# Normalising on VectorE instead of TensorE, finishing each down sum by halves, three tanh units begun at once, and the last stores on two queues, in a fused attention and two-layer feed-forward kernel on one core

## The chip, the cores and the metric

One core of one Trainium2 chip runs the kernel. The metric is device time in microseconds (us). Three runs of the kernel before gave 1197.57 us as median (1196.62 to 1197.73). Engines are named as in the profile: PE is TensorE (PEld its weight loads), DVE VectorE, ACT ScalarE, POOL GpSimd, SP SyncE; SPq and ACTq are the queues from which those engines issue transfers.

## The reference

6016 tokens of 256 channels go through a channel attention and two feed-forward layers.

```python
qn = q / (norm(q, axis=1) + 1e-6);  kn = k / (norm(k, axis=1) + 1e-6)
a = softmax(kn.T @ qn / tau)                 # 256 x 256, sums over all tokens
x = v @ a                                    # 6016 x 256
xn = x / sqrt(mean(x * x, axis=-1) + 1e-6) * rms_g
g, val = xn @ w_gate, xn @ w_val             # 256 -> 1536
y = (g * sigmoid(g) * val) @ w_out           # 1536 -> 256
h = y @ w_in                                 # 256 -> 2048
out = (h - tanh(h)) @ w_out2                 # 2048 -> 256
```

## The kernel before, in words

A first part streams q and k through PE in pieces of rows, builds the 256 x 256 attention matrix and normalises it. Then come twelve tiles of 512 tokens, the last of 384. Everything in a tile is kept with channels on the 128 partitions and tokens along the row. Tile 0 is written out by itself, tiles 1 to 9 are a hardware loop, tiles 10 and 11 are written out again.

Every fp32 factor is split into a rounded high part and a low rest, so one product is three matmuls (`PASSES`, L302): high by high, high by low, low by high. A tile has two stages. The first has G = 12 gated units of 128 hidden channels: gate and value are made by `up` (six matmuls each: two halves c of the 256 inputs by three passes), ACT applies the sigmoid, DVE multiplies twice (L718, L721), rounds (L819) and takes the rest (L731, result `h_lo`), and `down` adds the unit into the two halves d of `y_acc` (again six matmuls). The second stage has H = 16 tanh units: one `up` each, ACT tanh (L480), DVE subtracts (L727), L819, L731, and `down` adds into `out_acc`.

PE's order is written by hand (L964 to L1007). A unit's `down` comes LAG = 3 units behind its `up`; behind the last `up` of a stage stand four `down`s in a row (24 matmuls): one from the loop and three from the loop at L986 or L1006. Each `down` waits for `h_ready`, which `h_lo` counts. The matmul results of `up` go through a ring of four PSUM banks. At the end of a stage ACT copies `y_acc` rounded into `y_hi` (L501) and DVE makes `y_lo` (L738), half by half: half 0 may start at `y_full`, which is counted when half 0's last matmul is done, three matmuls before the stage's end (L955), half 1 when all is done. The first tanh unit waits for half 0 and then for half 1 (`y_ready`). In tiles 1 to 10 the next tile's x is made in between (`make_x`, twelve matmuls, L991); in tile 0 and in the last tile nothing stands there.

The norm of the next tile's x is made along the tanh units, by a table of unit numbers (L38, `next_x` L741): squares added (L584), transposed by blocks of 32 (L589), reduced (L593, giving `sums`, 128 x 16, where each quadrant of 32 partitions holds a part of each token's sum), the four quadrants added by one matmul with the constant matrix `quads` (`add_quads`, L919), the root on ACT (L424), the reciprocal and its spreading on DVE (L599, L601). In tile 0 the first x is normalised while PE already computes the first three gated units from x without the norm (`raw_gate`, `raw_value`, L755 to L766); there `add_quads` stands inside the first value unit (`sum_first`, L959), and everything DVE does next waits for it through ACT's root.

`quads` is filled by POOL (L396 to L402) behind its share of the weight splitting; `CONSTANTS` counts that fill, and DVE waits for it at L668 before it turns the norms of q and k into reciprocals (L671). Behind that stand the softmax and tile 0. PE runs matmuls without use at two places there (`warm_up`, L1009).

The results are transposed by DVE (L621, one instruction for each half of the channels) and stored by eight transfers per tile from SPq, four for each half (`store`, L337). ACTq is used for three loads at the start only (L432).

Of the kernel before, what the change touches and what calls it, by code (L numbers as in the profile page):

```python
# [5 lines left out]
F32 = mybir.dt.float32  # L6
# [5 lines left out]
P = 128  # L12
# [3 lines left out]
LAG = 3  # L16
RING = 4
# [18 lines left out]
SUM_AT = 4  # L36
SQRT_AT = 5
X_ADD, X_TURN, X_REDUCE, X_RMS, X_SCALE, X_CAST, X_SPLIT = 0, 1, 2, 6, 7, 9, 10  # L38
# [12 lines left out]
def build(nc, q, k, v, tau, w_gate, w_value, w_down, w_up2, w_down2, rms_g, out):  # L51
# [62 lines left out]
    with ExitStack() as ctx:  # L114
# [9 lines left out]
        quads = sb("quads", [P, P], F32)  # L124
# [34 lines left out]
        sums = sb("sums", [P, TILE // SQ], F32)  # L159
        rms = sb("rms", [P, TILE // SQ], F32)  # L160
# [37 lines left out]
        token_sums = y_acc[:, 0, 0:TILE // SQ]  # L198
# [36 lines left out]
        sum_step = sem("sum_step")  # L235
        sums_full = sem("sums_full")
# [16 lines left out]
        stored = sem("stored")  # L253

# [55 lines left out]
        def _(sp):  # L310
# [60 lines left out]
            sp.wait_ge(stored, TILE_DMAS * TILES)  # L371
# [3 lines left out]
        def _(pool):  # L375
# [20 lines left out]
            nc.gpsimd.memset(quads[:], 0.0).then_inc(constants, 1)  # L396
            for n in range(2 * QUADS - 1):

                pool.wait_ge(constants, 4 + n)
                nc.gpsimd.affine_select(out=quads[:], in_=quads[:], compare_op=ALU.not_equal, fill=1.0,  # L400
                                        base=(n - (QUADS - 1)) * SQ, pattern=[[-1, P]],
                                        channel_multiplier=1).then_inc(constants, 1)  # L402


        @block.scalar
        def _(act_e):
# [15 lines left out]
            def root(t, width):  # L422
                act_e.wait_ge(sums_full, t + 1)
# [135 lines left out]
            tile(TILES - 1, True)  # L559


        @block.vector
        def _(dve):
# [27 lines left out]
            def reduce_squares(t, width):  # L591
# [3 lines left out]
                                        AX_X, ALU.add).then_inc(sum_step, 1)  # L595

# [71 lines left out]
            dve.wait_ge(constants, CONSTANTS)  # L668
# [42 lines left out]
            reduce_squares(0, TILE)  # L711
            spread_scales(0, TILE)
# [28 lines left out]
            def next_x(t, f, ahead):  # L741
# [4 lines left out]
                if f == X_REDUCE:  # L746
                    reduce_squares(t + 1, ahead)
                if f == X_RMS:
                    spread_scales(t + 1, ahead)
# [98 lines left out]
        def _(pe):  # L848
# [70 lines left out]
            def add_quads(t, width):  # L919

                pe.wait_ge(sum_step, t * SUM_STEPS + SUM_STEPS)
                nc.tensor.matmul(token_sums[:, 0:width // SQ], quads[:, :], sums[:, 0:width // SQ],  # L922
                                 start=True, stop=True).then_inc(sums_full, 1)

            def tile(t, first, last):
# [3 lines left out]
                def up(name, weights, hi, lo, made=None, between=None):  # L929

                    free_bank(t, name)
                    for c in range(KC):
                        if made is not None:
                            pe.wait_ge(*made(c))
                        if c > 0 and between is not None:
                            between()
                        for w_part, part in PASSES:
                            ins = nc.tensor.matmul(bank(name)[:, 0:width], weights(c, w_part),  # L938
                                                   (hi if part else lo)[:, c, 0:width],
                                                   start=c == 0 and w_part and part,  # L940
                                                   stop=c == KC - 1 and not w_part)
                    ins.then_inc(bank_full, 1)

                def down(kind, f, u, units, acc, full):

                    if first and f % (BLOCK // C) == 0:
                        pe.wait_ge(w_ready, place[(kind, f // (BLOCK // C))] + 1)
                    pe.wait_ge(h_ready, t * U + (u + 1))
                    for d in range(KC):
                        for w_part, part in PASSES:  # L950
                            ins = nc.tensor.matmul(acc[:, d, 0:width], down_weight(kind, f, d, w_part),  # L951
                                                   (h_hi if part else h_lo)[:, u % RING, 0:width],
                                                   start=f == 0 and w_part and part,
                                                   stop=f == units - 1 and not w_part)
                        if f == units - 1 and d == 0:  # L955
                            ins.then_inc(full, 1)
                    ins.then_inc(h_used, 1)

                def sum_first():  # L959
                    pe.wait_ge(constants, CONSTANTS)  # L960
                    pe.wait_ge(x_copied, KC)
                    add_quads(0, TILE)

                for f in range(G):  # L964
# [3 lines left out]
                    for which, name in ((0, "gate"), (1, "value")):  # L968
# [3 lines left out]
                        if f == (RAW_UNITS if first else 0):  # L972
                            made = lambda c: (x_ready, t * KC + (c + 1))
                        up((name, f), lambda c, part: gv_weight(which, f, c, part),
                           u_hi if raw_unit else x_hi, u_lo if raw_unit else x_lo, made,
                           sum_first if first and (name, f) == ("value", 0) else None)

                    for late in ((), (0, 1))[f == LAG + 1] if first and f <= LAG + 1 else (f - LAG,):
                        if late < 0:
                            continue  # L980
                        if late == 0:
                            pe.wait_ge(rms_ready, t + 1)
                            if not first:
                                pe.wait_ge(y_ready, t * KC)
                        down("down", late, late, G, y_acc, y_full)
                for f in range(G - LAG, G):  # L986
                    down("down", f, f, G, y_acc, y_full)
# [4 lines left out]
                for f in range(H):  # L992
# [80 lines left out]
```

## Time and profile before

| | value |
|---|---|
| median of 3 runs | 1197.57 us |
| the profiled execution | 1195.46 us |
| its span (first to last instruction) | 1193.3 us |
| granted TensorE clock, mean | 0.998 |
| busy: PE, PEld | 99%, 83% |
| busy: DVE, ACT, POOL | 71%, 31%, 2% |
| chain that ended last: PE's share | 95% |

The span is what the trace covers; the rest of the execution's time lies around it. Busy shares are of the span. The chain that ended last goes back from the last instruction to whatever released it. PE's matmuls are pipelined: the listed duration of one (0.39 us) holds its way through the array, and the next starts some 0.23 us after it.

### The profile page before, as it was taken

Reading aid. Unit: us, or ns where it says so; the run is one execution under the profiler, and the core shown is the slowest. Engines: PE = TensorE matmul, PEld = TensorE weight load, DVE = VectorE, ACT = ScalarE, POOL = GpSimd, SP = SyncE. Lnnn points to the kernel's source line nnn. Section 1 sums busy time; section 2 is a strip of 40 time slices with the busy share of each in tenths; the row PEclk is TensorE's granted clock in tenths of the full one; section 3 lists DMA queues with packets and bytes.
Section 4 is the critical chain, followed back from the end, with each engine's and each line's share of the span. In section 5 each row is a group of like instructions: output and inputs, shape, how many; then the busy total and the mean of one; then the engine's idle time right before and its main releaser. Section 6 shows DMA issues by size and latency. Waiting matters only on the chain.

```text
span 1193.3 us, 15914 instructions
## 1 busy us (share of the span) xinstructions
PE 1179.2 (99%) x5339; PEld 986.0 (83%) x5339; DVE 845.0 (71%) x1375; ACT 365.9 (31%) x587; POOL 29.3 (2%) x27
## 2 busy tenths in 40 slices
PE   8999999999999999999999999999999999999998
PEld 7777888888888888888888888888888888888997
DVE  5697766866767677586596676766767758658665
ACT  6765621411321322231231141142132123123121
POOL 4400000000000000000000000000000000000000
PEclk9999999999999999999999999999999999999999
DMA  9515011011002002002001101100200100100100
GB/s 344 211 62 151 1 18 18 1 18 18 0 2 33 0 0 35 0 0 35 0 0 18 18 0 18 18 0 0 35 0 0 31 0 0 18 1 1 18 1 14
DMA packets 105210, 33.92 MB, mean 28 GB/s; under 512 B 92384, under 2 KB 100832, under 8 KB 105184
## 3 DMA queue, kind: packets, MB, share of 16 engines
q1 hardware_dynamic: 104752, 33.05, 11.0%
q10 hardware_dynamic: 432, 0.52, 0.1%
q8 instruction: 16, 0.26, 0.1%
q14 instruction: 10, 0.08, 0.0%
HBM read 27.40 MB, written 6.16 MB: 28 GB/s over the span
## 4 chain that ended last, share of the span: by engine, by line
PE 95%; DMA 2%; DVE 1%; POOL 1%; ACT 0%; SPq 0%; issue 0%; POOLq 0%; DVEq 0%; ACTq 0%
PE ring L938 54%; PE out_acc L951 21%; PE y_acc L951 16%; PE out_acc L909 2%; DMA qk_in<-in_q_dram 2%; PE y_acc L855 1%; PE y_acc L866 1%; POOL we_lo L393 0%; SPq L319 0%; PE y_acc L922 0%; PE y_acc L909 0%; POOL quads L400 0%; ACT y_hi L471 0%; DVE y_lo L738 0%; PE out_acc L1031 0%
## 5 line engine op out<-in xcount | busy, mean ns | idle before, releaser
L480 ACT ACTIVATE act<-ring 128x512 f32<-128x512 f32 (+1 forms) x333 | 196.5, 590 | 715.4 <-PE ring L938 698.9
L731 DVE TENSOR_TENSOR h_lo<-act,h_hi 128x512 fp32r<-128x512 f32 (+1 forms) x336 | 228.6, 680 | 10.7
L727 DVE TENSOR_TENSOR act<-ring,act 128x512 f32<-128x512 f32 (+1 forms) x192 | 129.2, 673 | 99.3 <-ACT act L480 99.2
L718 DVE TENSOR_TENSOR act<-ring,act 128x512 f32<-128x512 f32 (+1 forms) x141 | 94.9, 673 | 140.9 <-ACT act L480 140.9
L938 PE MATMUL ring<-y_hi,wl_hi 128*128 128x512 f32 (+1 forms) x384 | 148.8, 388 | 1.7 <-DVE y_lo L738 1.7
L938 PE MATMUL ring<-y_lo,wl_hi 128*128 128x512 f32 (+1 forms) x384 | 147.8, 385 | 0.0
L938 PE MATMUL ring<-y_hi,wl_lo 128*128 128x512 f32 (+1 forms) x384 | 147.7, 385 | 0.0
L951 PE MATMUL out_acc<-h_hi,wl_hi 128*128 128x512 f32 (+1 forms) x384 | 147.6, 384 | 0.0
L951 PE MATMUL out_acc<-h_lo,wl_hi 128*128 128x512 f32 (+1 forms) x384 | 147.6, 384 | 0.0
L951 PE MATMUL out_acc<-h_hi,wl_lo 128*128 128x512 f32 (+1 forms) x384 | 147.6, 384 | 0.0
L819 DVE CAST h_hi<-act 128x512 fp32r<-128x512 f32 (+1 forms) x308 | 129.8, 421 | 12.9
L938 PE MATMUL ring<-x_hi,wl_hi 128*128 128x512 f32 (+1 forms) x288 | 110.7, 384 | 0.0
L938 PE MATMUL ring<-x_lo,wl_hi 128*128 128x512 f32 (+1 forms) x288 | 110.7, 384 | 0.0
L938 PE MATMUL ring<-x_hi,wl_lo 128*128 128x512 f32 (+1 forms) x288 | 110.7, 384 | 0.0
L721 DVE TENSOR_TENSOR act<-ring,act 128x512 f32<-128x512 f32 (+1 forms) x141 | 95.9, 680 | 15.4
L938 PE MATMUL ring<-x_hi,we_hi 128*128 128x512 f32 (+1 forms) x276 | 106.2, 385 | 0.1
L938 PE MATMUL ring<-x_lo,we_hi 128*128 128x512 f32 (+1 forms) x276 | 106.1, 384 | 0.0
L938 PE MATMUL ring<-x_hi,we_lo 128*128 128x512 f32 (+1 forms) x276 | 106.1, 384 | 0.0
L938 PEld LDWEIGHTS ring<-y_hi,wl_hi 128*128 128x128 f32 x384 | 72.1, 188 | 15.8 <-issue 2.4
L951 PEld LDWEIGHTS out_acc<-h_hi,wl_hi 128*128 128x128 f32 x384 | 72.1, 188 | 14.0 <-DVE h_lo L731 0.2
L938 PEld LDWEIGHTS ring<-y_hi,wl_lo 128*128 128x128 f32 x384 | 72.1, 188 | 13.8
L951 PEld LDWEIGHTS out_acc<-h_hi,wl_lo 128*128 128x128 f32 x384 | 72.1, 188 | 13.7
(156 smaller groups left out, 1596.7 us busy)
## 6 DMA issues: line engine op xcount, KB each, us to landing
out_dram<-out_rows SPq DMA_DIRECT2D x88, 64.0 KB, 1.8
qk_in<-in_k_dram SPq DMA_DIRECT2D x9, 512.0 KB, 9.6
qk_in<-in_q_dram SPq DMA_DIRECT2D x9, 512.0 KB, 10.4
v_in<-in_v_dram SPq DMA_DIRECT2D x72, 64.0 KB, 2.2
w_in<-in_moe_w_out_dram SPq DMA_DIRECT2D x14, 256.0 KB, 2.9
w_in<-in_moe_w_in_dram SPq DMA_DIRECT2D x8, 256.0 KB, 3.2
w_in<-in_moe_w_gate_dram SPq DMA_DIRECT2D x6, 256.0 KB, 6.3
w_in<-in_moe_w_val_dram SPq DMA_DIRECT2D x6, 256.0 KB, 7.1
```

The costliest lines, as they stand in the source:

```text
L480: nc.scalar.activation(act[:, u % RING, 0:width], bank(name)[:, 0:width], func).then_inc(act_ready, 1)
L718: nc.vector.tensor_tensor(buf, bank(gate)[:, 0:width], buf, ALU.mult).then_inc(bank_free, 1)
L721: nc.vector.tensor_tensor(buf, bank(value)[:, 0:width], buf, ALU.mult).then_inc(bank_free, 1)
L727: nc.vector.tensor_tensor(buf, bank(hidden)[:, 0:width], buf, ALU.subtract).then_inc(bank_free, 1)
L731: nc.vector.tensor_tensor(h_lo[:, u % RING, 0:width], act[:, u % RING, 0:width], f32(h_hi[:, u % RING, 0:width]), ALU.subtract).then_inc(h ...
L819: nc.vector.tensor_copy(h_hi[:, slot, 0:width], act[:, slot, 0:width]).then_inc(h_hi_ready, 1)
L855: ins = nc.tensor.matmul(raw[:, m, 0:C], qk_in[:, stage, 0, j, m * P:(m + 1) * P], qk_in[:, stage, 1, j, :], start=i == 0 and j == 0, stop ...
L866: ins = nc.tensor.matmul(raw[:, m, 0:C], (qk_hi if k_part else qk_lo)[:, s % SLOTS, 0, j, m * P:(m + 1) * P], (qk_hi if q_part else qk_lo) ...
L909: ins = nc.tensor.matmul(acc[:, d, 0:width], (a_hi if a_part else a_lo)[:, c, d * P:(d + 1) * P], (hi if v_part else lo)[:, c, 0:width], s ...
L938: ins = nc.tensor.matmul(bank(name)[:, 0:width], weights(c, w_part), (hi if part else lo)[:, c, 0:width], start=c == 0 and w_part and part ...
L951: ins = nc.tensor.matmul(acc[:, d, 0:width], down_weight(kind, f, d, w_part), (h_hi if part else h_lo)[:, u % RING, 0:width], start=f == 0 ...
```

## The change

Four things are changed.

1. The four quadrants' partial sums are added by DVE. `quads`, POOL's fill of it and PE's `add_quads` go; DVE gets a function of that name with two adds of 64 partitions and four of 32, whose second input lies in another quadrant than the first. In tile 0 it stands behind the reduce, in the others behind the tanh unit of number 3 (`X_QUADS`). The softmax on DVE then waits for `ident` only.
2. The last three `down`s of each stage are done half by half: half 0 of all three units, then half 1 (`finish_down`).
3. In tile 0 and in the last tile the first three tanh units are begun together: half 0 of the inputs for all three, then half 1 (`hidden_units`, `HIDDEN_BEGUN`). In tiles 1 to 10 it is one unit, as before.
4. The last half of the last tile is stored by two transfers from SPq and two from ACTq.

```diff
-SUM_AT = 4
-X_ADD, X_TURN, X_REDUCE, X_RMS, X_SCALE, X_CAST, X_SPLIT = 0, 1, 2, 6, 7, 9, 10
+X_ADD, X_TURN, X_REDUCE, X_QUADS, X_RMS, X_SCALE, X_CAST, X_SPLIT = 0, 1, 2, 3, 6, 7, 9, 10
...
@@ store (SP) @@
-                    for quad in range(QUADS):
+
+                    shared = isinstance(t, int) and t == TILES - 1 and half == KC - 1
+                    for quad in range(QUADS // 2 if shared else QUADS):
...
@@ scalar @@
-                act_e.wait_ge(sums_full, t + 1)
+                act_e.wait_ge(sums_full, (t + 1) * QUADS)
...
+            act_e.wait_ge(out_turned, TILES * KC)
+            for quad in range(QUADS // 2, QUADS):
+                act_e.dma_start(tokens(out, TILES - 1, SHORT, KC - 1, quad),
+                                out_rows[quad * SQ:(quad + 1) * SQ, KC - 1, 0:SHORT // SQ, :]).then_inc(stored_last, 16)
@@ vector @@
+            def add_quads(t, width):
+
+                dve.wait_ge(sum_step, t * SUM_STEPS + SUM_STEPS)
+                for a in range(2):
+                    here, there = slice(a * 2 * SQ, (a + 1) * 2 * SQ), slice((1 - a) * 2 * SQ, (2 - a) * 2 * SQ)
+                    nc.vector.tensor_tensor(pair_sums[here, 0:width // SQ], sums[here, 0:width // SQ],
+                                            sums[there, 0:width // SQ], ALU.add).then_inc(pairs_ready, 1)
+                dve.wait_ge(pairs_ready, (t + 1) * 2)
+                for a in range(QUADS):
+                    here, there = slice(a * SQ, (a + 1) * SQ), slice((a ^ 1) * SQ, ((a ^ 1) + 1) * SQ)
+                    nc.vector.tensor_tensor(token_sums[here, 0:width // SQ], pair_sums[here, 0:width // SQ],
+                                            pair_sums[there, 0:width // SQ], ALU.add).then_inc(sums_full, 1)
...
-            dve.wait_ge(constants, CONSTANTS)
+            dve.wait_ge(constants, IDENT)
@@ tensor @@
+                def down_half(kind, f, d, u, units, acc):
+                    for w_part, part in PASSES:
+                        ins = nc.tensor.matmul(acc[:, d, 0:width], down_weight(kind, f, d, w_part),
+                                               (h_hi if part else h_lo)[:, u % RING, 0:width],
+                                               start=f == 0 and w_part and part,
+                                               stop=f == units - 1 and not w_part)
+                    return ins
...
+                def finish_down(kind, u, units, acc, full):
+
+                    for f in range(units - LAG, units):
+                        pe.wait_ge(h_ready, t * U + (u + f + 1))
+                        ins = down_half(kind, f, 0, u + f, units, acc)
+                    ins.then_inc(full, 1)
+                    for f in range(units - LAG, units):
+                        down_half(kind, f, 1, u + f, units, acc).then_inc(h_used, 1)
+
+                def hidden_units(units):
+
+                    for f in units:
+                        free_bank(t, ("hidden", f))
+                    for c in range(KC):
+                        pe.wait_ge(y_ready, t * KC + (c + 1))
+                        for f in units:
+                            up_half(("hidden", f), c, lambda c, part: up2_weight(f, c, part), y_hi, y_lo)
...
-                for f in range(G - LAG, G):
-                    down("down", f, f, G, y_acc, y_full)
+                finish_down("down", 0, G, y_acc, y_full)
...
+                begun = HIDDEN_BEGUN if first or last else 1
+                hidden_units(range(begun))
+                for f in range(begun, H):
...
-                    if f == SUM_AT and not last:
-                        add_quads(t + 1, ahead)
-                for f in range(H - LAG, H):
-                    down("down2", f, G + f, H, out_acc, out_full)
+                finish_down("down2", G, H, out_acc, out_full)
```

PE at the end of the second stage of the loop (tiles 1 to 9), before: the units numbered 14 and 15, from the rows that follow unit 13's `down`. `out_acc` is the sum of the stage, `wl_hi` and `wl_lo` the weight parts.

```order
L948 REGISTER_ALU
L951 MATMUL out_acc<-h_hi,wl_hi 128x512 [waits h_ready]
L951 MATMUL out_acc<-h_lo,wl_hi 128x512
L951 MATMUL out_acc<-h_hi,wl_lo 128x512
L951 MATMUL out_acc<-h_hi,wl_hi 128x512
L951 MATMUL out_acc<-h_lo,wl_hi 128x512
L951 MATMUL out_acc<-h_hi,wl_lo 128x512
L948 REGISTER_ALU
L951 MATMUL out_acc<-h_hi,wl_hi 128x512 [waits h_ready]
L951 MATMUL out_acc<-h_lo,wl_hi 128x512
L951 MATMUL out_acc<-h_hi,wl_lo 128x512
L951 MATMUL out_acc<-h_hi,wl_hi 128x512
```

And PE there now, from the first of the three last units (13) on.

```order
L975 REGISTER_ALU
L958 MATMUL out_acc<-h_hi,wl_hi 128x512 [waits h_ready]
L958 MATMUL out_acc<-h_lo,wl_hi 128x512
L958 MATMUL out_acc<-h_hi,wl_lo 128x512
L975 REGISTER_ALU
L958 MATMUL out_acc<-h_hi,wl_hi 128x512 [waits h_ready]
L958 MATMUL out_acc<-h_lo,wl_hi 128x512
L958 MATMUL out_acc<-h_hi,wl_lo 128x512
L975 REGISTER_ALU
L958 MATMUL out_acc<-h_hi,wl_hi 128x512 [waits h_ready]
L958 MATMUL out_acc<-h_lo,wl_hi 128x512
L958 MATMUL out_acc<-h_hi,wl_lo 128x512
```

Before, six matmuls stood between the wait for one unit and the wait for the next; now three do. The nine matmuls of half 1 follow behind these rows.

PE at the start of the last tile's tanh units, before: the first unit's two halves with their waits for `y_ready`, then the second unit.

```order
L938 MATMUL ring<-y_hi,wl_hi 128x384 [waits y_ready,bank_free]
L938 MATMUL ring<-y_lo,wl_hi 128x384
L938 MATMUL ring<-y_hi,wl_lo 128x384
L938 MATMUL ring<-y_hi,wl_hi 128x384 [waits y_ready]
L938 MATMUL ring<-y_lo,wl_hi 128x384
L938 MATMUL ring<-y_hi,wl_lo 128x384
L938 MATMUL ring<-y_hi,wl_hi 128x384 [waits bank_free]
L938 MATMUL ring<-y_lo,wl_hi 128x384
L938 MATMUL ring<-y_hi,wl_lo 128x384
```

And now: half 0 of three units, then the wait for half 1.

```order
L942 MATMUL ring<-y_hi,wl_hi 128x384 [waits bank_free,y_ready]
L942 MATMUL ring<-y_lo,wl_hi 128x384
L942 MATMUL ring<-y_hi,wl_lo 128x384
L942 MATMUL ring<-y_hi,wl_hi 128x384
L942 MATMUL ring<-y_lo,wl_hi 128x384
L942 MATMUL ring<-y_hi,wl_lo 128x384
L942 MATMUL ring<-y_hi,wl_hi 128x384
L942 MATMUL ring<-y_lo,wl_hi 128x384
L942 MATMUL ring<-y_hi,wl_lo 128x384
L942 MATMUL ring<-y_hi,wl_hi 128x384 [waits y_ready]
L942 MATMUL ring<-y_lo,wl_hi 128x384
L942 MATMUL ring<-y_hi,wl_lo 128x384
```

Three matmuls stood between the wait for half 0 and the wait for half 1; now nine do, and the first unit is complete after twelve instead of six.

DVE in tile 0, before, from the adding of the squares to the spreading of the reciprocals.

```order
L584 TENSOR_TENSOR vt<-vt 128x512 [waits sq_ready]
L589 STREAM_TRANSPOSE scales<-vt 128x512 [waits sum_step]
L593 TENSOR_REDUCE sums<-scales 128x16 [waits sum_step]
L599 RECIPROCAL rrms<-rms 128x16 [waits rms_ready]
L601 STREAM_TRANSPOSE scales<-rrms 128x512 [waits scale_step]
```

And now, with two rows more at the end.

```order
L585 TENSOR_TENSOR vt<-vt 128x512 [waits sq_ready]
L590 STREAM_TRANSPOSE scales<-vt 128x512 [waits sum_step]
L594 TENSOR_REDUCE sums<-scales 128x16 [waits sum_step]
L603 TENSOR_TENSOR pair_sums<-sums 64x16 [waits sum_step]
L603 TENSOR_TENSOR pair_sums<-sums 64x16
L608 TENSOR_TENSOR token_sums<-pair_sums 32x16 [waits pairs_ready]
L608 TENSOR_TENSOR token_sums<-pair_sums 32x16 x3
L613 RECIPROCAL rrms<-rms 128x16 [waits rms_ready]
L615 STREAM_TRANSPOSE scales<-rrms 128x512 [waits scale_step]
```

Six adds now stand ahead of the reciprocal, and ACT's root waits for the last of them.

SP's last rows before: each half of the last tile is one transfer that waits and three more.

```order
L341 DMA out_0_dram<-out_rows 32x16x32 [waits out_turned]
L341 DMA out_0_dram<-out_rows 32x16x32 x3
L341 DMA out_0_dram<-out_rows 32x12x32 [waits out_turned]
L341 DMA out_0_dram<-out_rows 32x12x32 x3
L341 DMA out_0_dram<-out_rows 32x12x32 [waits out_turned]
L341 DMA out_0_dram<-out_rows 32x12x32 x3
L114 UNCONDITIONAL_BRANCH [waits stored]
```

And now.

```order
L345 DMA out_0_dram<-out_rows 32x16x32 [waits out_turned]
L345 DMA out_0_dram<-out_rows 32x16x32 x3
L345 DMA out_0_dram<-out_rows 32x12x32 [waits out_turned]
L345 DMA out_0_dram<-out_rows 32x12x32 x3
L345 DMA out_0_dram<-out_rows 32x12x32 [waits out_turned]
L345 DMA out_0_dram<-out_rows 32x12x32
L114 UNCONDITIONAL_BRANCH [waits stored_last,stored]
```

Two of the eight are gone from here; they stand at the end of ACT's program, behind its last tanh, and wait for the same transpose.

## Rows read from the trace of the kernel before

**Rows 1.** The page: busy time of the engines.
```profile
PE 1179.2 (99%) x5339; PEld 986.0 (83%) x5339; DVE 845.0 (71%) x1375; ACT 365.9 (31%) x587; POOL 29.3 (2%) x27
```
**Rows 2.** Busy time in the stretch of one tile of the loop.
```profile
159.46:255.16 95.70, 95.70 (x424) 78.98 (x423) 68.07 (x111) 25.14 (x42) 0.00 (x0) 1.00 0.07 12
```
**Rows 3.** The chain that ended last, in order of time: start, us, what.
```profile
219.46 1.36 PE out_acc L951 x6
220.82 0.38 PE y_acc L922 x2
221.20 1.48 PE ring L938 x6
...
1081.54 0.12 PE y_acc L922 x2
```
**Rows 4.** Instructions in order: start, duration, engine; last `up` matmul, last `h_lo`, loop tile.
```profile
249.49 0.39 PE L938 MATMUL ring<-y_hi,wl_lo 128*128 128x512 f32 x1
...
251.90 0.69 DVE L731 TENSOR_TENSOR h_lo<-act,h_hi 128x512 fp32r<-128x512 f32 x1
```
**Rows 5.** The same view, tile 0: PE released by an `h_lo`.
```profile
79.25 0.68 DVE L731 TENSOR_TENSOR h_lo<-act,h_hi 128x512 fp32r<-128x512 f32 x1
...
79.98 0.50 PE L951 MATMUL y_acc<-h_hi,we_hi 128*128 128x512 f32 x1
```
**Rows 6.** The same, first stage's end, loop tile: last `h_lo`, last of 24 matmuls.
```profile
204.62 0.69 DVE L731 TENSOR_TENSOR h_lo<-act,h_hi 128x512 fp32r<-128x512 f32 x1
...
208.19 0.39 PE L951 MATMUL y_acc<-h_hi,wl_lo 128*128 128x512 f32 x1
```
**Rows 7.** The same, ahead of the softmax; in brackets idle time and what ended it.
```profile
52.57 0.17 ACT L456 ACTIVATE norms<-out_acc 128x4 f32<-128x4 f32 x1 [2.11 <-PE out_acc L895]
...
53.83 0.16 DVE L671 SCALAR_TENSOR_TENSOR norms<-norms,tau 128x4 f32<-128x4 f32 x1 [3.36 <-POOL quads L400]
...
52.40 1.91 PE L1012 MATMUL ring<-vt_hi 128*128 128x512 f32 x4
54.78 1.22 PE L1031 MATMUL out_acc<-act,ones 128*128 128x256 f32 x2 [0.47 <-DVE act L676]
```
**Rows 8.** The same, the first norm in tile 0.
```profile
65.89 0.69 DVE L593 TENSOR_REDUCE sums<-scales 128x16 f32<-128x512 f32 x1
...
67.12 0.27 ACT L424 ACTIVATE rms<-y_acc,eps 128x16 f32<-128x16 f32 x1 [1.37 <-PE y_acc L922]
...
67.43 0.25 DVE L599 RECIPROCAL rrms<-rms 128x16 f32<-128x16 f32 x1 [0.86 <-ACT rms L424]
...
81.72 0.50 PE L938 MATMUL ring<-x_hi,we_hi 128*128 128x512 f32 x1
```
**Rows 9.** The same, tile 0 between its stages.
```profile
111.66 0.68 DVE L731 TENSOR_TENSOR h_lo<-act,h_hi 128x512 fp32r<-128x512 f32 x1
...
115.53 0.47 PE L938 MATMUL ring<-y_hi,wl_hi 128*128 128x512 f32 x1 [0.88 <-DVE y_lo L738]
...
119.80 0.68 DVE L731 TENSOR_TENSOR h_lo<-act,h_hi 128x512 fp32r<-128x512 f32 x1
...
121.08 0.39 PE L951 MATMUL out_acc<-h_hi,wl_hi 128*128 128x512 f32 x1
```
**Rows 10.** The same, last tile: its first tanh unit, its last `h_lo`.
```profile
1154.06 0.41 PE L938 MATMUL ring<-y_hi,wl_hi 128*128 128x384 f32 x1 [0.80 <-DVE y_lo L738]
...
1185.00 0.56 DVE L731 TENSOR_TENSOR h_lo<-act,h_hi 128x384 fp32r<-128x384 f32 x1
```
**Rows 11.** The last stores and the first loads of ACTq; the last wait.
```profile
1187.12 1.11 DVE L621 STREAM_TRANSPOSE out_rows<-out_acc 128x384 f32<-128x384 f32 x2 [1.57 <-PE out_acc L951]
1187.73 3.90 SPq L341 DMA_DIRECT2D out_dram<-out_rows  x8
...
0.74 1.39 ACTq L432 DMA_DIRECT2D qk_in<-in_q_dram  x3
...
SPq L114 <- DMA out_dram<-out_rows: 1.3, 1, 1.3
```

More of the change, by code:

```diff
@@ L16 @@
 LAG = 3
+HIDDEN_BEGUN = 3
 RING = 4
@@ L747, in next_x @@
                     reduce_squares(t + 1, ahead)
+                if f == X_QUADS:
+                    add_quads(t + 1, ahead)
                 if f == X_RMS:
@@ L927, in tile, with up_half, up @@
                 ahead = width_of(t + 1)
-                def up(name, weights, hi, lo, made=None, between=None):
+                def up_half(name, c, weights, hi, lo):
+                    for w_part, part in PASSES:
+                        ins = nc.tensor.matmul(bank(name)[:, 0:width], weights(c, w_part),
+                                               (hi if part else lo)[:, c, 0:width],
+                                               start=c == 0 and w_part and part,
+                                               stop=c == KC - 1 and not w_part)
+                    if c == KC - 1:
+                        ins.then_inc(bank_full, 1)
+                def up(name, weights, hi, lo, made=None):
                     free_bank(t, name)
@@ L934, in up, with down @@
                             pe.wait_ge(*made(c))
[L935 to L944, printed above, removed]
+                        up_half(name, c, weights, hi, lo)
+                def down_half(kind, f, d, u, units, acc):
+                    for w_part, part in PASSES:
+                        ins = nc.tensor.matmul(acc[:, d, 0:width], down_weight(kind, f, d, w_part),
[3 more added lines that the diff above has]
+                    return ins
+                def down(kind, f, u, units, acc):
                     if first and f % (BLOCK // C) == 0:
@@ L949, in down @@
                     for d in range(KC):
[L950 to L956, printed above, removed]
-                    ins.then_inc(h_used, 1)
[L959 to L962, printed above, removed]
+                        ins = down_half(kind, f, d, u, units, acc)
+                    ins.then_inc(h_used, 1)
+                def finish_down(kind, u, units, acc, full):
[12 more added lines that the diff above has]
+                            up_half(("hidden", f), c, lambda c, part: up2_weight(f, c, part), y_hi, y_lo)
                 for f in range(G):
@@ L981, in tile @@
                         if late == 0:
-                            pe.wait_ge(rms_ready, t + 1)
-                            if not first:
+                            if first:
+                                pe.wait_ge(x_copied, KC)
+                            else:
                                 pe.wait_ge(y_ready, t * KC)
-                        down("down", late, late, G, y_acc, y_full)
-                for f in range(G - LAG, G):
-                    down("down", f, f, G, y_acc, y_full)
+                        down("down", late, late, G, y_acc)
+                finish_down("down", 0, G, y_acc, y_full)
                 if not last and not first:
@@ L991, in tile @@
                     make_x(x_acc, vt_hi, vt_lo, ahead, WHOLE_X)
-                for f in range(H):
+                if first:
+                    pe.wait_ge(w_ready, place[("up2", 0)] + 1)
+                begun = HIDDEN_BEGUN if first or last else 1
+                hidden_units(range(begun))
+                for f in range(begun, H):
                     if first and f % (BLOCK // KC // P) == 0:
                         pe.wait_ge(w_ready, place[("up2", f // (BLOCK // KC // P))] + 1)
-                    up(("hidden", f), lambda c, part: up2_weight(f, c, part), y_hi, y_lo,
-                       (lambda c: (y_ready, t * KC + (c + 1))) if f == 0 else None)
+                    up(("hidden", f), lambda c, part: up2_weight(f, c, part), y_hi, y_lo)
                     if f >= LAG:
```

26 lines of the change are left out of this document (9 added, 17 removed).

## Prediction

> **What bounds the kernel.** I read the page's busy times first: PE is busy for 99% of the span [rows 1]. So only what leaves PE's own stream, or what holds it at its few gaps, can move the time. The stretch of one loop tile says more: PE is busy through all of its 95.70 us with 424 matmuls, at a granted clock of 1.00, that is 2.4 GHz [rows 2]. The chain of waits in order of time gives the price of a matmul: six take 1.36 us, 0.2267 each [rows 3]. 420 such matmuls are 95.20 us; the remaining 0.50 us of a tile belongs to the four records that are not of that kind or that stand beside it, and the chain names them: 0.38 us for the sum over the quadrants and 0.12 more in the six behind it (1.48 for 1.36) [rows 3]. DVE is busy for 68 of the 95.70 us and has room. The rest of the loop has no gap at all. Gaps are left ahead of the softmax, in tile 0, between the stages of tile 0 and of the last tile, and behind the last matmul.
>
> **Part 1, the sum over the quadrants, tiles 1 to 10.** The sum for the next tile leaves PE in each: nine times 0.50 us in the loop, and about 0.24 in tile 10 (0.12 and the same 0.12 behind it) [rows 3]: -4.7 us. On DVE six small adds come in. No row shows an add of 32 or 64 partitions with inputs in different quadrants. The nearest are 0.16 us (128x4) and 0.25 us (reciprocal, 128x16) [rows 7, 8]; I take 0.18 each, 1.1 us in all, with ends at 0.6 and 1.5. They are hidden there: they stand behind unit 3, and DVE has 27 us of room in a tile. What waits for them is ACT's root at unit 5, two units (5.4 us) later, and unit 4's `h_lo`, whose `down` comes three units behind its `up`. Without this cover they would cost their own 1.1 us per tile.
>
> **Part 1 in tile 0 and ahead of the softmax.** DVE's first step of the softmax starts at 53.83, idle 3.36 us on POOL's fill; the roots from ACT were there at 52.74 [rows 7]. That is 1.0 us to take back, but next is PE: its four useless matmuls end at 54.31, some 0.15 of which is the way through the array, so its matmul at 54.78 can start at 54.15 [rows 7]. Gain 0.6 us. It is spent at once: before, ACT's root started 0.54 us after the reduce (66.58 to 67.12) [rows 8], now 1.1 us of adds lie between. Everything DVE does from there runs without a break until it releases PE at 81.72 [rows 8], so that moment stays: 0.0 us, with ends -0.6 (adds at 0.10 each) and +0.5. The 0.6 us that PE loses at the sum itself in tile 0 isn't a gain, for the same chain holds it later.
>
> The Trainium skill, "VectorE: DVE Perf Modes", section "Two Vector instructions with no wait between them", speaks here: an instruction whose inputs or output start in another quadrant than those of the one in front is held until all earlier ones have finished. All six adds would be held by it, and the sum above, with 0.18 each, is in effect by that rule; without it they would overlap, at about 0.10 us apart, and the total would be -4.0 instead of -3.5. No row of before has two such instructions.
>
> **Part 2, the finish by halves, end of the second stage.** This is the term that works against the change. Before, the last tanh unit's first `down` matmul stood in the 19th slot behind the last `up`; now it is the 13th. In the loop the last `up` matmul starts at 249.49, so the 13th slot is 249.72 + 12 x 0.2267 = 252.44. The unit's `h_lo` ends at 251.90 + 0.69 = 252.59 [rows 4]. What a late `h_lo` costs beyond that is seen in tile 0: it ended at 79.93, PE went on at 79.98, and that matmul took 0.50 instead of 0.39 [rows 5], so 0.16 us more. PE stalls 252.59 + 0.16 - 252.44 = 0.31 us. The chain ahead of it (ACT's tanh, then three steps of DVE) hangs on the `up` itself and doesn't come earlier. Ten tiles (1 to 10): +3.1 us, with ends 0 (the wait lies in time that PE has anyway) and +6 (0.6 each, when the restart is as slow as the gap in rows 9 with its 0.47 start).
>
> End of the first stage: `h_lo` ends at 205.31; the last of the 24 matmuls starts at 208.19, the 13th eleven slots before it, at 205.70 [rows 6]. 0.39 us of room, less 0.16: costs nothing in the loop, and the earlier half 0 of y wins nothing there, for twelve matmuls of the next x lie between the stages.
>
> **Tile 0.** There the last gated unit's `h_lo` ends only at 112.34, because ACT and DVE split a weight block in between [rows 9]. The last of the 24 matmuls before starts about at 114.3 (115.53 less the idle 0.88 and the way through the array), the 13th slot at 111.8: a stall of 0.7. In exchange the second stage starts as soon as the first ends, near 115.3 instead of 115.53, and runs without the slow start. Its first `down` stood at 121.08, its `h_lo` was ready at 120.48 [rows 9]. Now unit 0 is complete six matmuls later and ACT, which first takes the next x, is about 0.9 us later; `h_lo` 0 comes at about 121.3, `down` at 121.45: +0.4. The sum on PE is gone (-0.5). The lateness of ACT and DVE with two further weight blocks, and the root that waits for the adds while ACT has two table loads around it, I estimate at +0.4, and the stage's end at +0.3. Tile 0: +0.6 us, ends -0.5 and +1.5.
>
> **Part 3, last tile.** The idle 0.80 us at its first tanh unit [rows 10] goes, with some 0.2 of slow start: half 0 of y is counted nine matmuls ahead of the end instead of three, and nine matmuls of half 0 cover the making of half 1. -1.0. Late next is unit 0 of the tanh units, complete only twelve matmuls ahead of its `down`, the same distance as at a stage's end: +0.3; and the stage's end, where `h_lo` at 1185.56 [rows 10] comes about as late as in the loop: +0.2. Together -0.5, ends -1.1 and 0.
>
> **Part 4, the last stores.** Eight issues take 3.90 us, 0.49 each, from 1187.73; SP then waits 1.3 us for the last to land [rows 11]. Now half 0 is full six matmuls earlier (6 x 0.17 = 1.0 us): SP starts at 1186.7, its four are out at 1188.65. Half 1 is full at 1187.65, turned at 1188.2; SP's two end at 1189.6, ACTq's two (0.46 each [rows 11]) at 1189.2. The last issue ends 2.0 us earlier than 1191.63. -2.0, ends -1.0 (if landing, not issuing, limits) and -2.2. ACT has nothing queued behind its two.
>
> **Sum.** -4.7 + 0.0 + 3.1 + 0.6 - 0.5 - 2.0 = -3.5 us. The profiled execution took 1195.46 (span 1193.3 and 2.16 around it), so it would be 1192.0; the median of the runs lies 2.1 above that execution, so the forecast is 1197.57 - 3.5 = 1194.1. Within 0.2% means within 2.4 us, about what a measurement of this kernel can tell from no change.
>
> **Rivals.** (A) The finish by halves costs nothing: -3.1 and the like terms in tiles 0 and 11 fall away, 1190.5. For it: `h_lo` is late by only 0.15 us against the slot. Against: the restart in rows 5. 12%. (B) The finish costs more: every stage's end waits 0.5 to 0.6 us, or tile 0 is at its upper end: the gain shrinks to 1 us, 1196.6. For it: the chain of four steps has no slack, and two units may be late, not one. 17%. (C) Stores overlap less and tile 0 is slower, each at its end: 1195.6. 7%. (D) Slower: the adds across quadrants on DVE are much dearer than any small row. They start to hold PE when ACT's root is late for unit 6, or unit 4's `h_lo` for its `down`: about 3.1 us of adds per tile, 0.5 each. At 0.7 each (4.2 us) PE loses about 1.1 us in each of eleven tiles and 3.1 more in tile 0: 1194.1 + 12 + 3 = 1209. Against: 0.16 to 0.25 us in the rows. 5%. (E) The change doesn't do what it says: the wait ahead of the softmax moves to another releaser and the norm in tile 0 comes later, with no gain from either; at most 1 us, inside the forecast.
>
> **Chances.** The forecast's own case (gain of 2.4 to 5 us) 59%, A 12%, B 17%, C 7%, D 5%. Faster by over 0.2%: 59 + 12 less a little of the forecast's edge, 0.69. Within: B and C and that edge, 0.25. Slower: 0.06. Range 1190.8 to 1196.7: A and B at its edges.
>
> **What would show it.** In a loop tile: 422 matmuls, no quadrant sum, a length of 95.5 us instead of 95.70; a gap or a slow matmul of about 0.3 us at the 13th matmul behind the last `up`, released by `h_lo`; none in the first stage. Six DVE adds of about 0.18 us, each starting when the last has ended. DVE's first softmax step near 52.8, PE's at 54.15, and PE released at 81.7 as before. In tile 0 a gap of 0.7 near 111.8. In the last tile no gap at the first tanh unit but one of 0.3 at its first `down`. The last issue 2.0 us nearer to the last matmul. Wrong if a loop tile takes 95.2 us (A) or 95.7 and more (B), or if an add takes over 0.5 us (D).

## The result and the profile after

The changed kernel takes 1193.62 us (median of 12 runs, 1191.94 to 1196.03); the kernel before took 1197.65 us in the 12 runs beside them. The ratio is 0.9970, 95% interval 0.9961 to 0.9978, so 3.6 us less, between 2.6 and 4.7 (the two medians lie 4.0 apart). The forecast was 3.5 us less, at 1194.1.

The page of the profiled execution (1193.26 us), its head and the engines' busy times:

```profile
span 1191.3 us, 15906 instructions
PE 1179.2 (99%) x5315; PEld 983.2 (83%) x5315; DVE 855.7 (72%) x1447; ACT 366.4 (31%) x587; POOL 27.1 (2%) x19
```

24 matmuls fewer and 72 DVE instructions more than in [rows 1]; PE stays the bound. The stretch of one loop tile, the counterpart of [rows 2]:

```profile
160.99:256.53 95.54, 95.48 (x421) 78.75 (x420) 68.99 (x117) 25.17 (x42) 0.00 (x0) 1.00 0.07 12
```

95.54 us instead of 95.70. Instructions in order of time at the end of its second stage, which answer to [rows 4] (start, duration, engine, line, operation):

```profile
250.52 0.39 PE L942 MATMUL ring<-y_hi,wl_lo 128*128 128x512 f32 x1
...
252.94 0.69 DVE L746 TENSOR_TENSOR h_lo<-act,h_hi 128x512 fp32r<-128x512 f32 x1
...
253.68 0.50 PE L958 MATMUL out_acc<-h_hi,wl_hi 128*128 128x512 f32 x1
254.02 0.40 PE L958 MATMUL out_acc<-h_lo,wl_hi 128*128 128x512 f32 x1
```

The 13th slot behind the last `up` matmul was 250.75 + 12 x 0.2267 = 253.47. `h_lo` ends at 253.63, PE goes on at 253.68 and its matmul is 0.11 us longer in the array than its neighbours, as in [rows 5]. The tile loses 0.34 us here, of the 0.50 that it gained by the missing sum.

Ahead of the softmax and in tile 0 (compare [rows 7] and [rows 8]), the same view:

```profile
53.14 0.17 DVE norms L685
...
54.09 1.22 PE out_acc L1056 x2
55.31 3.30 PE ring L1037 x11
```

These three are pieces of the chain of waits. DVE no longer waits for POOL. But the chain now runs over the eleven useless matmuls (L1037), where before it ran over DVE. Next the six adds, in order of time:

```profile
65.48 0.69 DVE L594 TENSOR_REDUCE sums<-scales 128x16 f32<-128x512 f32 x1
66.20 0.37 DVE L603 TENSOR_TENSOR pair_sums<-sums 64x16 f32<-64x16 f32 x2
66.61 0.76 DVE L608 TENSOR_TENSOR token_sums<-pair_sums 32x16 f32<-32x16 f32 x4
67.74 0.25 DVE L613 RECIPROCAL rrms<-rms 128x16 f32<-128x16 f32 x1 [0.37 <-ACT rms L421]
```

They take 1.17 us, 0.20 from one to the next. Then the two longest waits of PE in tile 0 behind its release by DVE, which were not there before, and a third, for the unit behind ACT's root:

```profile
112.73 0.50 PE L958 MATMUL y_acc<-h_hi,wl_hi 128*128 128x512 f32 x1 [0.47 <-DVE h_lo L746]
...
121.77 0.47 PE L958 MATMUL out_acc<-h_hi,wl_hi 128*128 128x512 f32 x1 [0.58 <-DVE h_lo L746]
...
135.99 0.50 PE L958 MATMUL out_acc<-h_hi,wl_hi 128*128 128x512 f32 x1 [0.15 <-DVE h_lo L746]
```

The end, which answers to [rows 10] and [rows 11]:

```profile
1157.73 0.41 PE L958 MATMUL out_acc<-h_hi,wl_hi 128*128 128x384 f32 x1 [0.17 <-DVE h_lo L746]
...
1186.53 2.90 SPq L345 DMA_DIRECT2D out_dram<-out_rows  x6
...
1187.10 0.34 PE L958 MATMUL out_acc<-h_hi,wl_lo 128*128 128x384 f32 x1
1187.48 0.58 DVE L635 STREAM_TRANSPOSE out_rows<-out_acc 128x384 f32<-128x384 f32 x1 [0.98 <-PE out_acc L958]
1188.09 0.87 ACTq L559 DMA_DIRECT2D out_dram<-out_rows  x2
```

The last tile has no gap at its first tanh unit any more, a small one at that unit's first `down`; the row of six issues on SPq begins 0.57 us before the last matmul, and the two on ACTq run beside its end.

To put the executions side by side I measured stretches between marks that all of them have, from the start times of PE's matmuls. The first mark is the first one-column matmul of the norms (50.62 us before, 50.88 after), for the loads ahead of it end at different times from run to run. "Release" is the gate unit for which DVE frees the bank (81.72 before). The spans end at 1193.345 and 1191.315.

| stretch, us | before | after | change | forecast |
|---|---|---|---|---|
| first column matmul to release | 31.10 | 31.16 | +0.1 | 0.0 |
| release to tile 1 | 77.74 | 78.95 | +1.2 | +0.6 |
| tiles 1 to 10 | 956.17 | 954.75 | -1.4 | -1.6 |
| last tile, to its last matmul | 71.64 | 71.36 | -0.3 | -0.5 |
| last matmul to the end of the span | 6.07 | 4.21 | -1.9 | -2.0 |

The sum is -2.3, with the 0.26 us of the first mark -2.0, as the spans say (1193.3 and 1191.3).

### The profile page after: what moved, and what is told of

It reads as the page before. It is cut to its first block, busy times and chain, and to the rows that moved or that the text cites. A ratio compares the mean times of both kernels' runs of the same rounds, so it can differ in the third digit from the quotient of the medians.

```text
span 1191.3 us, 15906 instructions
## 1 busy us (share of the span) xinstructions
PE 1179.2 (99%) x5315; PEld 983.2 (83%) x5315; DVE 855.7 (72%) x1447; ACT 366.4 (31%) x587; POOL 27.1 (2%) x19
## 4 chain that ended last, share of the span: by engine, by line
PE 89%; DVE 5%; ACT 2%; DMA 2%; issue 1%; SPq 0%; DVEq 0%; ACTq 0%
PE ring L942 51%; PE out_acc L958 18%; PE y_acc L958 16%; PE out_acc L926 2%; DMA qk_in<-in_q_dram 2%; DVE h_lo L746 1%; DVE act L742 1%; ACT act L477 1%; PE y_acc L872 1%; DVE h_hi L836 1%; PE y_acc L883 1%; DVE wl_lo L580 0%; SPq L321 0%; PE ring L1037 0%; PE y_acc L926 0%
```

## The experiments

The theory: the sum over the quadrants gives 0.50 us back in each tile, the finish by halves takes 0.34 of it away at the second stage's end, tile 0 pays for late units, and the stores give about 2 us. The rivals: the halves cost nothing and the tile is bound elsewhere; or the adds on DVE are what takes the gain away.

In the kernels below `finish_down` takes the number of units done by halves (1 is the order of before), from a table of six: both stages of tile 0, of tiles 1 to 10 and of the last tile; `BEGUN` has the tanh units begun in each of the three.

```diff
-                def finish_down(kind, u, units, acc, full):
-
-                    for f in range(units - LAG, units):
+                def finish_down(kind, u, units, acc, full, depth):
+                    for f in range(units - LAG, units - max(depth, 1)):
+                        down(kind, f, u + f, units, acc)
+                    for f in range(units - max(depth, 1), units):
```

**The adds alone.** Whole `down`s, one tanh unit begun, and the stores as before:

```diff
-HIDDEN_BEGUN = 3
+BEGUN = (1, 1, 1)
+FINISH = (1, 1, 1, 1, 1, 1)
...
-                    for quad in range(QUADS // 2 if shared else QUADS):
+                    for quad in range(QUADS):
```

> Only the quadrant adds move to VectorE; whole downs, one tanh unit and eight stores on one queue as before. Theory (PE's slot is given back in full): a loop tile 95.20 us instead of 95.70, tile 0 about 0.3 us later at the point where VectorE releases TensorE near 81.7, ten tiles -4.7; in all -4.4 us against before. Rival (the adds hold h_lo, and TensorE loses there what it gains): a loop tile 95.5 or more and no more than -2 us.

Measured: 1191.77 us (1191.62 to 1192.30), ratio to before 0.9955, interval 0.9941 to 0.9968. The chain of waits, first stretch of tile 1 and of tile 2:

```profile
160.88 10.88 PE ring L938 x48
...
256.08 10.88 PE ring L938 x48
```

95.20 us for the tile, so the 0.50 us come back in full and the adds hold nothing there. The release comes 0.3 us later than before, as expected, and from release to tile 1 it takes 78.03 us, 0.3 more than before: the adds push ACT's root in tile 0. By the ratio the time falls by 5.4 us (3.8 to 7.1), where 4.4 were expected; the stretches of the trace add to 4.1. By the ratios this part alone beats the whole change by 1.8 us; the two intervals overlap, but the same stretches of the two traces add to 1.9.

**Halves in the last tile only.**

```diff
-HIDDEN_BEGUN = 3
+BEGUN = (3, 1, 3)
+FINISH = (1, 1, 1, 1, 3, 3)
```

> The changed kernel with whole downs in tiles 0 to 10 and halves only in the last tile. Theory (halves cost 0.34 us at the end of the second stage of each tile): a loop tile 95.20 us instead of the 95.54 of the changed kernel, no wait for h_lo there, 3.0 to 3.5 us faster than the changed kernel and 6 to 7 faster than before. Rival (the slow matmul there is a mere shift of records, tiles are bound elsewhere): tile stays 95.5 and the time within 1 us of the changed kernel.

Measured: 1189.80 us (1189.30 to 1191.26), ratio 0.9940 (0.9926 to 0.9953).

```profile
160.96 10.88 PE ring L943 x48
...
256.15 10.88 PE ring L943 x48
```

95.19 us. 3.8 us less than the changed kernel's median, 3.6 by the ratios to before (the two were not timed in one series). In the traces the halves' price is 3.3 us, all of it in tiles 1 to 10 (951.43 us against 954.75); from release to tile 1 it takes 78.98 us against 78.95, so in tile 0 leaving the halves out wins nothing while three tanh units are begun.

**Two units by halves**, at all stages' ends.

```diff
-HIDDEN_BEGUN = 3
+BEGUN = (3, 1, 3)
+FINISH = (2, 2, 2, 2, 2, 2)
```

> The changed kernel with two units by halves instead of three at every stage's end. Theory: the last unit's h_lo is then needed three slots (0.68 us) later, more than the 0.31 us by which it is late, so a loop tile is 95.20 us as with whole downs; 3 to 4 us faster than the changed kernel; in tile 0 and the last tile half 0 of y comes a little late (0.2 to 0.4 us of wait at the first tanh unit). Rival (any splitting by halves costs, through the order of weights or the extra waits): 95.4 to 95.5 us.

Measured: 1190.27 us (1190.01 to 1191.16), ratio 0.9943 (0.9929 to 0.9956).

```profile
160.77 10.88 PE ring L943 x48
...
255.97 10.88 PE ring L943 x48
```

95.20 us: it isn't the splitting that costs, it is how early the last unit is wanted. With two it is wanted in the 16th slot, and `h_lo` is there. Half 0 of y comes late, as expected: PE waits 0.17 us at the first tanh unit of tile 0, and the last tile takes 71.54 us against 71.36.

**Four units by halves** in the second stage of tiles 1 to 10, the same in the other direction; the loop over the units then leaves out its last `down`.

```diff
-HIDDEN_BEGUN = 3
+BEGUN = (3, 1, 3)
+FINISH = (3, 3, 3, 4, 3, 3)
```

> The changed kernel with four units by halves at the end of the second stage of tiles 1 to 10, so the last unit's h_lo is needed three slots (0.68 us) earlier still. Theory (each slot earlier is a slot of stall): the stall grows from 0.34 to 1.02 us and a loop tile takes 96.2 us instead of 95.54. Rival (stall is a fixed cost of the halves' order): 95.54.

Measured: 1200.66 us, one run. The chain, and then the stall in order of time:

```profile
161.80 10.88 PE ring L943 x48
...
258.03 10.88 PE ring L943 x48
```

```profile
254.33 0.50 PE L959 MATMUL out_acc<-h_hi,wl_hi 128*128 128x512 f32 x1 [0.73 <-DVE h_lo L747]
```

96.23 us for the tile. With two, three and four units it takes 95.20, 95.54 and 96.23: from three to four one unit's three slots (0.68 us) are added in full. This settles the mechanism of this term.

**One tanh unit begun**, with the halves of the changed kernel.

```diff
-HIDDEN_BEGUN = 3
+BEGUN = (1, 1, 1)
+FINISH = (3, 3, 3, 3, 3, 3)
```

> The changed kernel with one tanh unit begun in tile 0 and the last tile as before. Theory: half 0 of y is in time, but half 1 is ready only about 1.95 us after its last matmul started, so the first unit waits some 1.0 us between its halves (0.9 in the last tile), while its first down comes without the 0.6 us wait of the changed kernel in tile 0: tile 0 about 0.3 us longer and the last tile 0.5 to 0.9 longer than in the changed kernel. Rival (three units bring nothing beside the halves): both tiles equal or shorter.

Measured: 1193.96 us, one run. PE's waits in order of time, in tile 0 and in the last tile:

```profile
117.19 0.50 PE L943 MATMUL ring<-y_hi,wl_hi 128*128 128x512 f32 x1 [0.79 <-DVE y_lo L754]
...
1154.72 0.44 PE L943 MATMUL ring<-y_hi,wl_hi 128*128 128x384 f32 x1 [0.71 <-DVE y_lo L754]
```

Release to tile 1 takes 79.09 us against 78.95, the last tile 71.95 against 71.36. So beside the halves three units are worth 0.6 us in the last tile and only 0.1 in tile 0 (0.3 was expected), where the wait moves to the first `down`. Over the 78.03 us of quads_only, halves alone cost tile 0 1.06 us, three units alone 0.95 (no_halves_loop) and both together 0.92.

**The stores alone**, on the kernel before: SPq issues two of the last four, ACTq two.

```diff
-                    for quad in range(QUADS):
+                    shared = isinstance(t, int) and t == TILES - 1 and half == KC - 1
+                    for quad in range(QUADS // 2 if shared else QUADS):
```

> The kernel before with the last half's four stores shared between two queues. Theory: SP's sixth issue ends about 1.0 us earlier than its eighth did, so the distance from the last matmul's start to the end of the span goes from 6.03 to 5.05 us and the time by -1.0 us; the other 0.8 of the changed kernel's tail came from the earlier first half. Rival (landing limits): under 0.3 us.

Measured: 1196.03 us (11 runs), ratio 0.9990 (0.9981 to 0.9999).

```profile
1188.56 0.34 PE L958 MATMUL out_acc<-h_hi,wl_lo 128*128 128x384 f32 x1
...
1189.02 2.92 SPq L343 DMA_DIRECT2D out_dram<-out_rows  x6
1189.55 0.87 ACTq L565 DMA_DIRECT2D out_dram<-out_rows  x2
```

From the last matmul to the end of the span (1193.65) 5.09 us instead of 6.07: -1.0, as expected and as two issues of 0.49 us make it. The changed kernel has 4.21 there; the other 0.9 are the earlier half 0. Issuing limits, not landing.

**Adds that all start in the first quadrant.**

```diff
-                    nc.vector.tensor_tensor(pair_sums[here, 0:width // SQ], sums[here, 0:width // SQ],
-                                            sums[there, 0:width // SQ], ALU.add).then_inc(pairs_ready, 1)
+                    nc.vector.tensor_tensor(pair_sums[:, cols], sums[:, cols],
+                                            sums[:, cols], ALU.add).then_inc(pairs_ready, 1)
```

> The changed kernel, but its six small adds all cover 128 partitions, start in the first quadrant and add a few columns to themselves (8 and 4 columns in place of 16), so the sum over the quadrants is left out. Theory (an instruction whose inputs or output start in another quadrant than the one in front is held until all earlier ones ended): the adds then stand about 0.10 to 0.13 us apart instead of 0.20. Rival (0.20 us is the least distance of any small add on VectorE): they stay at 0.19 to 0.20.

The loop tile's adds, in order of time (one run, 1192.60 us):

```profile
223.17 0.23 DVE L604 TENSOR_TENSOR pair_sums<-sums 128x8 f32<-128x8 f32 x2
223.44 0.38 DVE L610 TENSOR_TENSOR token_sums<-pair_sums 128x4 f32<-128x4 f32 x4
223.74 0.68 DVE L744 TENSOR_TENSOR act<-ring,act 128x512 f32<-128x512 f32 x1
```

Four start within 0.30 us, 0.075 apart, where the changed kernel's stand 0.20 apart. Some 0.01 us of that I put down to the smaller number of columns, for one add takes 0.155 us instead of 0.165. So the 0.20 is not the least distance of small adds; changing the quadrant costs 0.12 us each. Which of the two does it, inputs in two quadrants or an output in another than the last, this kernel doesn't tell. The Trainium skill's rule on held instructions ("VectorE: DVE Perf Modes", "Two Vector instructions with no wait between them") agrees.

The same kernel prices the adds in tile 0, where they stand ahead of what ACT and DVE do for the next x. The adds and ACT's first tanh behind the root, in the changed kernel and then here:

```profile
127.91 0.76 DVE L608 TENSOR_TENSOR token_sums<-pair_sums 32x16 f32<-32x16 f32 x4
...
134.04 0.58 ACT L477 ACTIVATE act<-ring 128x512 f32<-128x512 f32 x1
```

```profile
127.34 0.38 DVE L610 TENSOR_TENSOR token_sums<-pair_sums 128x4 f32<-128x4 f32 x4
...
132.97 0.58 ACT L477 ACTIVATE act<-ring 128x512 f32<-128x512 f32 x1
```

The release lies 0.32 us earlier here, the tanh 1.07. PE no longer waits at that unit's `down`, and from release to tile 1 it takes 78.46 us instead of 78.95: 0.5 us of tile 0's loss is the length of the adds (one run).

**A faster kernel.** Whole `down`s in the loop, halves of three in the last tile; in tile 0 two units by halves at the first stage's end and two tanh units begun; five adds:

```diff
-HIDDEN_BEGUN = 3
+BEGUN = (2, 1, 3)
+FINISH = (2, 1, 1, 1, 3, 3)
...
-                for a in range(2):
-                    here, there = slice(a * 2 * SQ, (a + 1) * 2 * SQ), slice((1 - a) * 2 * SQ, (2 - a) * 2 * SQ)
-                    nc.vector.tensor_tensor(pair_sums[here, 0:width // SQ], sums[here, 0:width // SQ],
-                                            sums[there, 0:width // SQ], ALU.add).then_inc(pairs_ready, 1)
+                nc.vector.tensor_tensor(pair_sums[low, 0:width // SQ], sums[low, 0:width // SQ],
+                                        sums[high, 0:width // SQ], ALU.add).then_inc(pairs_ready, 1)
...
-                    nc.vector.tensor_tensor(token_sums[here, 0:width // SQ], pair_sums[here, 0:width // SQ],
-                                            pair_sums[there, 0:width // SQ], ALU.add).then_inc(sums_full, 1)
+                    nc.vector.tensor_tensor(token_sums[here, 0:width // SQ], pair_sums[0:SQ, 0:width // SQ],
+                                            pair_sums[SQ:2 * SQ, 0:width // SQ], ALU.add).then_inc(sums_full, 1)
```

> Whole downs in the loop and halves of three only in the last tile, as in no_halves_loop; in tile 0 two units by halves at the first stage's end and two tanh units begun; five adds instead of six (one of 64 partitions, four of 32). Theory: loop tile 95.20; the adds in tile 0 take 0.20 us less on the path to TensorE's release; tile 0 from that release to its first down of the second stage 39.3 us instead of 40.1 (no_halves_loop) and 39.7 (changed kernel); 0.8 to 1.0 us faster than no_halves_loop, about -7.5 us against before. Rival (tile 0 is bound by ScalarE's take of the next x and not by the begun units): within 0.3 us of no_halves_loop.

Measured: 1189.02 us (1188.07 to 1190.37), ratio 0.9936 (0.9923 to 0.9950). From release to the first `down` of the second stage 38.84 us (39.3 expected), against 40.10 in no_halves_loop and 39.73 in the changed kernel; release to tile 1 77.48, a little better than before the change and 1.5 below no_halves_loop. Its median is 0.8 us below that of no_halves_loop, which was timed in another series; by the ratios it is 0.5, and the intervals overlap, so only the traces tell these two apart. What each of the three edits in tile 0 gives was not tried by itself.

**Fewer useless matmuls.** The same kernel with 7, and once more with 11 on the same chip.

```diff
-WARM_NORMS, WARM_SOFTMAX = 4, 11
+WARM_NORMS, WARM_SOFTMAX = 4, 7
```

> five_two_begun with 7 useless matmuls ahead of the first x instead of 11. Theory (with TensorE at 0.50 for some 3 us somewhere between 52 and 59 us, the 11 useless matmuls end later than VectorE's a_lo and hold the first x by 0.4 to 1.0 us): the first x starts when a_lo is there, about 6.7 us behind the first column matmul instead of 7.5, and the time falls by 0.4 to 0.8 us against five_two_begun. Rival (the slow stretch then falls on the matmuls of x and costs there what was saved): within 0.3 us of five_two_begun.

> The same kernel as five_two_begun, on the chip of best_seven_warm, for their comparison: 1189.0 us within 0.5, ratio to before 0.993 to 0.994.

Measured: 1187.99 us (1186.97 to 1189.93) with 7, 1188.72 (1187.17 to 1189.16) with 11; ratios to before 0.9921 (0.9908 to 0.9934) and 0.9923 (0.9910 to 0.9936). The chain with 11:

```profile
54.55 0.72 PE out_acc L1060 x2
55.27 4.09 PE ring L1041 x11
59.36 0.68 PE y_acc L926 x3
```

With 7, PE waits for DVE instead:

```profile
59.91 0.50 PE L926 MATMUL y_acc<-vt_hi,a_hi 128*128 128x512 f32 x1 [0.29 <-DVE a_lo L711]
```

From the first column matmul to the first x 7.15 us against 7.86, where 6.7 was expected: in these two traces most of the theory's gain is there. But five_two_begun, the same kernel as five_again, had 7.46, and the times can't tell 0.7 us apart, so it stays unclear.

## Why the prediction was right, step by step

**The sum over the quadrants** ([rows 3]): -0.50 us per loop tile, confirmed by the 95.20 us without halves. **The adds**: 0.18 us each were assumed, 0.20 measured; hidden in the loop, as said.

**The finish by halves**, loop: 0.31 us forecast from [rows 4] and [rows 5], 0.34 measured, and two more doses on the line. Rival A fell (the wait is real), B also (only one unit is late, and by little), and so did D: an add costs 0.20 us, not 0.5. Of C the half on tile 0 came (+1.2, its end was +1.5), the half on the stores did not. At the first stage's end no wait showed, as the 0.39 us of room in [rows 6] said.

**Ahead of the softmax**: PE's first matmul of the softmax came 3.21 us behind the first column matmul instead of 4.16, so 0.95 was won and not 0.6. The bound I used, PE's four useless matmuls ending at 54.31 [rows 7], was not a fixed one: they took 1.91 us there and 1.38 in the changed kernel, and the granted clock is why (next section). 0.43 of the gain went again in the eleven useless matmuls, a step that the prediction had not named: the first x comes 7.57 us behind the first column matmul instead of 8.09. From there to the reduce 0.15 us were won, and with the adds ACT's root starts 1.23 us behind the reduce instead of 0.54 (+0.69, forecast +0.56). The sum came out at 0.1, near the forecast for partly other reasons, and so in part by luck.

**Tile 0** is the term that was mis-sized: +0.6 forecast, +1.2 measured. Up to the first `down` of the second stage the forecast held: PE won 0.27 us between the stages (forecast 0.2) and lost 0.64 at the `down`, +0.37 together (forecast +0.4). What failed stands behind it: -0.5 for the missing sum, +0.4 for late units and +0.3 at the stage's end make +0.2, and it was +0.84. The sum had cost only 0.30 us there, not the 0.50 of a loop tile (3.02 us from one unit's `down` to the next instead of 2.72). On to unit 5 PE lost 0.33 us net, of which the adds alone make 0.14 (quads_only) and the three tanh units the rest; from there to tile 1 it lost 0.51, of which the adds make 0.12 and the halves 0.35 (25.00 us against 24.65 in no_halves_loop). The adds thus more than used up what the missing sum gave back: with adds that aren't held the 0.5 us return (adds_one_quadrant).

**Last tile**: -0.3 instead of -0.5; its gap went (0.97 us), its first `down` cost 0.26 (forecast 0.3), the stage's end and what stands before it 0.43 (forecast 0.2).

**Stores**: -1.9 for -2.0; the single parts, -1.0 and -0.9, fit.

The parts in the traces add to -2.3 us while the times say -3.6 (2.6 to 4.7). The profiled execution of before was 2.2 us below its own median, that of the changed kernel 0.4. Part of this goes with TensorE's clock: in 35 further executions of the kernel before its granted mean was 0.997 (0.995 to 1.000), in the 12 of the changed kernel 0.998, and both profiled executions have 0.998. A mean lower by 0.001 is 1.2 us of full clock lost in such a span, and the 10 executions of before with 0.996 or less took 1197.5 us at the median, the 7 with 0.998 or more 1196.3. So about 1 us of the 3.6 may be clock and not work that was removed; whether the change brought that about stays open. The forecast had added up to -3.5 from parts of which the traces show -2.3, so that the total agrees so closely is in part luck; the mechanisms of the loop and of the stores are not.

## What to carry to other kernels

Before a consumer is moved forward in a saturated engine's order, look up the producer's chain and count the slots: here 0.34 us of lateness and restart, at the end of eleven tiles, ate most of what a removed instruction had brought, and moving the demand back by three slots gave it all back. Changes that arrive together should be timed apart: the adds alone came out faster than the whole. A trick that helps where the pipe has a gap (last tile) should be switched on only there.

## What the runs showed of the hardware that I had not expected

TensorE's granted clock falls to its lower level (0.50, 1.2 GHz) for some 3.4 us around the softmax, behind matmuls of one column and a short gap, and where this falls differs between executions. Busy time by microsecond, before and then changed (the clock is the number behind POOL's):

```profile
52.00:53.00 1.00, 1.00 (x7) 0.90 (x8) 0.00 (x0) 0.41 (x2) 0.58 (x2) 0.78 0.99 333
53.00:54.00 1.00, 1.00 (x4) 0.48 (x2) 0.16 (x1) 1.00 (x1) 0.58 (x2) 0.50 0.42 145
54.00:55.00 1.00, 0.53 (x2) 0.23 (x2) 0.94 (x4) 0.72 (x3) 0.00 (x0) 0.50 0.00 0
55.00:56.00 1.00, 1.00 (x3) 0.82 (x4) 0.12 (x1) 0.00 (x0) 0.00 (x0) 0.51 0.00 0
56.00:57.00 1.00, 1.00 (x5) 0.83 (x5) 0.90 (x4) 0.31 (x1) 0.00 (x0) 1.00 0.00 0
```

```profile
53.00:54.00 1.00, 1.00 (x4) 0.35 (x2) 0.79 (x5) 0.98 (x2) 0.00 (x0) 0.72 0.60 209
54.00:55.00 1.00, 0.95 (x4) 0.82 (x3) 0.43 (x2) 0.87 (x3) 0.00 (x0) 0.50 0.00 0
55.00:56.00 1.00, 1.00 (x4) 0.72 (x4) 0.59 (x3) 0.00 (x0) 0.00 (x0) 0.50 0.00 0
56.00:57.00 1.00, 1.00 (x4) 0.81 (x3) 0.84 (x5) 0.94 (x3) 0.00 (x0) 0.57 0.00 0
57.00:58.00 1.00, 1.00 (x7) 0.79 (x6) 0.93 (x4) 1.00 (x3) 0.00 (x0) 1.00 0.02 8
```

Before, the stretch fell mostly on matmuls without use and on the gap behind them; in stores_only (56 to 59.4) and in the changed kernel it fell on the eleven useless matmuls and held the first x. In the profiled execution of no_halves_loop the clock stayed at 1.00, and the first x came 6.62 us behind the first column matmul instead of 7.46 to 8.83 in the other kernels with eleven useless matmuls. The two traces of one program, five_two_begun and five_again, have 7.46 and 7.86. So a single trace of this kernel is uncertain at its start by 0.4 us at the least, and by about 1 us if the whole spread is of this kind.
